# Attention, expert layer and gated layer on one core: expert stage and last stage in one block, idle matmuls in three waits of TensorE, and broadcasts of 1/rms behind the value share

## The chip, the cores and the metric

One core of one Trainium2 chip runs the whole program. Times are device microseconds of that core; a kernel's time is the median of its runs. TensorE, VectorE, ScalarE and GpSimd compute, SyncE (SP) issues the DMAs.

## The reference

```python
x = attention(q, k, v)              # 4 batches x 8 heads, 1152 queries pooled in pairs to 576, d 64
x = x.reshape(2304, 512)            # tokens
# expert layer with soft slots, 8 experts x 4 slots
logits = x @ phi                    # 2304 x 32
d = softmax(logits, over tokens);   slot_input = d.T @ x          # 32 x 512
slot_out[e] = relu(slot_input[e] @ w1[e]) @ w2[e]                 # 512 -> 1024 -> 512
c = softmax(logits, over slots);    x = c @ slot_out
# gated layer
xn = x / rms(x) * rms_g
out = (silu(xn @ w_gate) * (xn @ w_val)) @ w_out                  # 512 -> 1536 -> 512
```

All of it is fp32. The kernel never builds the x that enters the gated layer. It multiplies the 32 rows of `slot_out` by `w_gate` and `w_val` first (a share each of 32 x 1536) and then the softmax weights `c` by that. The factor 1/rms of each token is applied behind.

## The kernel before, in words

The program is four blocks one after another: attention, the routing of tokens to slots, the experts, the last stage. In a block each engine has its own list of instructions with semaphore waits written by hand; at the end of a block every engine, SP too, drains and meets the others.

**Routing** (lines 831 to 993). TensorE transposes x (L867), forms the logits (L877), transposes them back (L883, L886) and then waits for `col_exp`, the exponentials of the softmax over tokens: VectorE's maxima, one reduction over partitions by GpSimd, a subtraction by VectorE, the exponential by ScalarE (L918). Then come the weighted sums of x into `z_ps` (L892), the copy to `z_sum` (L922), a small product (L899) and `slot_in` (L988). VectorE prepares the inverse column sums meanwhile (L985).

**Experts** (lines 996 to 1188). Two groups of four experts, each expert in its own quarter of TensorE's columns. For a group: 32 matmuls into `h_ps` (L1103), relu by ScalarE, eight transposes, copies into `hid_t`, 32 matmuls into `o_ps` (L1139), a copy to `so_sb` (L1164), four transposes into `st_ps` (L1147), copies into `st_plain` (L1179) and, once, `st_scaled` (L1184). SP loads the second group's weights during the first: part c of `w1` when the part it overwrites has been used (`w1_used`, L1066), the four parts of `w2` behind (L1074), then `w_gv`, the weights of gate and value (L1079, L1081), and, when the second `o_ps` is complete, `w_out` into `wo_raw` in three issues (L1085). In the second group TensorE waits before every eighth of the 32 output matmuls for a part of `w2` (`w2_in[0]` to `w2_in[3]`). `stack_transposes` (L1034) writes the transposed softmax weights through `tb2`, and ScalarE copies them out (L1044, `ct_out`).

**Last stage** (lines 1193 to 1563). TensorE forms the Gram matrix of `st_plain` (L1304), ScalarE and VectorE split it into `gram_hi` and `gram`, TensorE multiplies the tokens by it (L1312, 20 matmuls of 32 columns), and VectorE and ScalarE make 1/rms from that (`inv_ready`). `share(m, c)` (L1259) adds part c to the share of gate (m = 0) or value (m = 1); `high_half` on ScalarE and `low_half` on VectorE split a share in two; `stack_share(k)` (L1273, L1275) puts quarter k of the eight into `tb3`, from which VectorE (even k) and ScalarE (odd k) copy it to `w_low`. `broadcast_inverse(n)` (L1282, L1287) spreads 1/rms of one batch (n = 0 to 3) or of the tails (4) over the partitions, in the PSUM bank `INV_BANK[n]`, and ScalarE copies it out (`inverse_out`, `bcast_out`). `gate` and `value` (L1296, L1300) make one tile of 128 hidden columns for 512 tokens; VectorE scales, ScalarE applies Silu (L1402), VectorE multiplies, and the product is split into `h_hi` (L1449) and `h_lo` (L1541). The loop over 5 chunks of tokens and 12 hidden tiles multiplies with the split `w_out` (L1364, three products per tile of tokens). `wo_hi` is made by ScalarE (L1381) and `wo_lo` by GpSimd (L1461), tile by tile ahead of the first chunk. The order of shares, broadcasts, gates and values ahead of this loop is written out by hand on TensorE and again on ScalarE (L1315 to L1345, L1404 to L1420). The accumulators `y_ps` of the loop are banks 4 to 7, so TensorE waits there for all broadcasts to be copied.

Of the kernel before, what the change touches and what calls it, by code (L numbers as in the profile page):

```python
# [6 lines left out]
P = 128  # L7
FP32 = mybir.dt.float32
F32R = mybir.dt.float32r
ALU = mybir.AluOpType  # L10
# [5 lines left out]
SQ = S // 2  # L16
# [745 lines left out]
def rest(nc, mem, phi, w1, w2, w_gate, w_val, w_out, rms_g, out):  # L762
# [95 lines left out]
    def _(pe):  # L858
# [28 lines left out]

        pe.wait_ge(col_exp, 1)
# [121 lines left out]
    tb2 = mem.ps("tb2", [P, 2, 512])  # L1010
# [44 lines left out]

    block = mem.block()
# [29 lines left out]

    @block.tensor
    def _(pe):
        for g in range(NG):
# [60 lines left out]
    @block.scalar  # L1150
    def _(act):
        for g in range(NG):
            act.wait_ge(h_ready, 2 * g + 1)
            if g:
                act.wait_ge(st_ready, g)
            nc.scalar.activation(hid[:, 0:512], h_ps[:, 0, :], ACT.Relu).then_inc(h_out, 1)
            act.wait_ge(h_ready, 2 * g + 2)
            nc.scalar.activation(hid[:, 512:1024], h_ps[:, 1, :], ACT.Relu).then_inc(h_out, 1)

            act.wait_ge(t_ready, 2 * g + 2)  # L1160
            if g:
                stack_out(act, tb2, plain_t)
            act.wait_ge(o_ready, g + 1)
            nc.scalar.copy(so_sb[:, 0:512], o_ps[:, :]).then_inc(o_out, 1)  # L1164

    @block.vector
    def _(dve):
        split_comb(dve)
        build_spread()
        for g in range(NG):  # L1170
            for n in range(2):
                dve.wait_ge(t_ready, 2 * g + n + 1)
                if g:
                    dve.wait_ge(o_ready, g)
                nc.vector.tensor_copy(hid_t[:, 4 * n:4 * n + 4, :],
                                      t_ps[:, n, :].rearrange("p (f q) -> p f q", f=4)).then_inc(t_out, 1)
            dve.wait_ge(st_ready, g + 1)
            for rep in range(4):
                last = nc.vector.tensor_copy(  # L1179
                    st_plain[:, :, rep, 16 * g:16 * g + 16].rearrange("p c (r s) -> p c r s", r=4),  # L1180
                    st_ps[:, :].rearrange("p (c r s) -> p c r s", c=KT, r=4)[:, :, :, 0:SPE])
            last.then_inc(st_out, 1)
        dve.wait_ge(st_out, NG)
        nc.vector.tensor_tensor(st_scaled[:], st_plain[:, :, 0, :],  # L1184
                                g_sb[:, :].unsqueeze(2).broadcast_to([P, KT, NS]), ALU.mult).then_inc(st_out, 1)
        dve.wait_ge(st_out, NG + 1)

    mem.end_block()

    mem.phase = mem.new_phase()
    QW = FF // 4
    N = NF * P
    CHUNKS = B + 1
    mem.at = r2
    w_low = mem.sb("w_low", [P, 2, FF], F32R)
    inv_rms = mem.sb("inv_rms", [P, NTOK], FP32)
    w_hi = mem.sb("w_hi", [P, 2, QW], F32R)  # L1200
    w_lo = mem.sb("w_lo", [P, 2, QW], F32R)
    assert mem.at <= r2 + 2 * SLOT
    mem.at = r2 + 4 * SLOT
    wo_hi = mem.sb("wo_hi", [P, NFT, DM], F32R)
    wo_lo = mem.sb("wo_lo", [P, NFT, DM], F32R)
    assert mem.at <= r3
    mem.at = r3
    scaled = mem.sb("scaled", [P, 2, N], FP32)
    silu = mem.sb("silu", [P, 2, N], FP32)
    hid2 = mem.sb("hid2", [P, 2, N], FP32)  # L1210
    h_hi = mem.sb("h_hi", [P, 3, N], F32R)
    h_lo = mem.sb("h_lo", [P, 3, N], F32R)
    y_sb = mem.sb("y_sb", [P, NF, DM], FP32)
    assert mem.at <= end_r3
    warm = hid[:, DM:DM + 2]

    banks = mem.ps("banks", [P, 8, 512])
    gv_ps = banks[:, 0:4, :].rearrange("p (f m) n -> p f m n", f=2)
    y_ps = banks[:, 4:8, :]
    g_ps = banks[:, 0, 0:NS]  # L1220
    gy_ps = banks[:, 2:4, :]
    w_ps = banks[:, 4:6, :]
    tb3 = banks[:, 6:8, :]
    INV_BANK = (1, 3, 4, 5, 4)

    gram_ready, gram_step, gy_ready = sem("gram_ready"), sem("gram_step"), sem("gy_ready")
    sq_step, mean_done, root, inv_ready = sem("sq_step"), sem("mean_done"), sem("root"), sem("inv_ready")
    bcast_ready, bcast_out = sem("bcast_ready"), sem("bcast_out")
    share_ready, share_hi, share_lo = sem("share_ready"), sem("share_hi"), sem("share_lo")
    wl_ready, wl_out_v, wl_out_a = sem("wl_ready"), sem("wl_out_v"), sem("wl_out_a")  # L1230
    wo_split_hi, wo_split_lo = sem("wo_split_hi"), sem("wo_split_lo")
    gate_ready, val_ready = sem("gate_ready"), sem("val_ready")
    scaled_done, silu_done, hid_done = sem("scaled_done"), sem("silu_done"), sem("hid_done")
    hi_done, lo_done, y_ready, y_out_a, y_out_v = sem("hi_done"), sem("lo_done"), sem("y_ready"), sem("y_out_a"), sem("y_out_v")
    used, stored, tail_done = sem("used"), sem("stored"), sem("tail_done")
    block = mem.block()
    SHARES = [(m, j) for m in range(2) for j in range(4)]

    def width_of(n):
        return N if n < B else TAIL * B  # L1240

    def columns(n):
        return slice(N * n, N * n + width_of(n))

    def tiles_of(n):
        return width_of(n) // P

    def row_scale(n, t):
        return tok_a[:, B * t + n:B * t + n + 1] if n < B else tail_inv[:, t:t + 1]

    def shares_out_before(k):
        return (k + 1) // 2, k // 2

    @block.tensor
    def _(pe):
# [83 lines left out]
        stack_share(6)  # L1339
        pe.wait_ge(bcast_out, 3)  # L1340
        broadcast_inverse(4)
        stack_share(7)
# [29 lines left out]
    def _(act):  # L1372

# [37 lines left out]
        inverse_out(1)  # L1411
        gate_silu(0)
        gate_silu(1)
        inverse_out(2)
        high_half(1)
        share_out(5)
        inverse_out(3)
        wo_high((0,))
        inverse_out(4)
# [21 lines left out]
        for n in range(CHUNKS):  # L1441
            width = width_of(n)
            for f in range(NFT):
# [22 lines left out]
    def _(dve):  # L1466
        dve.wait_ge(gram_step, 1)
# [79 lines left out]

    @block.sync
    def _(sp):
        o_rows = out.rearrange("(b s) d -> b s d", b=B)  # L1550
        o_full = o_rows[:, 0:NF * P, :].rearrange("b (p i) d -> p b (i d)", i=NF)
        for n in range(B):
            sp.wait_ge(y_out_a, 2 * n + 2)
            sp.wait_ge(y_out_v, 2 * n + 2)
            sp.dma_start(o_full[:, n, :], y_sb[:, :, :].rearrange("p i d -> p (i d)")).then_inc(stored, 16)
        sp.wait_ge(y_out_a, 2 * B + 1)
        sp.wait_ge(y_out_v, 2 * B + 1)
        for b in range(B):
            rows = slice(TAIL * (b % 2), TAIL * (b % 2) + TAIL)
            sp.dma_start(o_rows[b, NF * P:SQ, :], y_sb[rows, b // 2, :]).then_inc(stored, 16)  # L1560
        sp.wait_ge(stored, 16 * (2 * B))
# [84 lines left out]
```

## Time and profile before

| | |
|---|---|
| median of 3 runs | 858.87 us (858.35 to 860.64) |
| the profiled execution's own time | 856.21 us |
| its span | 854.4 us |
| TensorE busy | 792.5 us (93%) |
| VectorE busy | 497.3 us (58%) |
| ScalarE busy | 462.2 us (54%) |
| mean granted TensorE clock | 0.98 of 2.4 GHz |
| moved by DMA | 114.39 MB |

A row of the timeline is the start in us, the duration, the engine, the line and operation, result and operands, shape and the number of records; in brackets stand the idle time before it and what ended it. An fp32 matmul stands as two records. A row of the windows is the stretch, its length, the busy time of TensorE (or of each engine), the granted clock as a share of 2.4 GHz, the DMA engines' busy share and the GB/s they moved. Overlapping records are merged in busy times.

### The profile page before, as it was taken

The numbers are of one execution on the slowest core, as the hardware profiler recorded it, in microseconds if no ns is written. First come the engines' busy times: TensorE is split into PE (matmuls) and PEld (weight loads), VectorE is DVE, ScalarE is ACT, GpSimd is POOL, SyncE is SP. The second block draws the span as 40 slices with busy tenths as digits, with TensorE's granted clock in tenths as the row PEclk, the third lists the DMA queues.
The fourth block names the chain that finished last, engine by engine and source line by source line (L and its number), as shares of the span: only waits on it lengthen the run. The fifth ranks groups of instructions, "written<-read, shape, count | busy, mean of one in ns | idle before, by whom it ended". The sixth has DMA issues, their size and how long they took to land. (4 is left out here: it accounts for less than half of the span.)

```text
span 854.4 us, 17186 instructions
## 1 busy us (share of the span) xinstructions
PE 792.5 (93%) x5701; PEld 603.7 (71%) x5701; DVE 497.3 (58%) x956; ACT 462.2 (54%) x888; POOL 171.2 (20%) x230
## 2 busy tenths in 40 slices
PE   1799999999999999999999999986956899999997
PEld 1677777777778777777777777762314688888885
DVE  3566666576676566666665766645101566666664
ACT  1566666666667667666676666621112554334332
POOL 1323314314224124133143130000000240000000
PEclk9999999999999999999999999998986999999999
DMA  8984383473563653743734529346997001010111
GB/s 215 285 196 99 98 195 79 117 172 77 138 144 81 162 111 90 186 95 98 191 78 117 138 53 290 130 166 238 401 399 290 2 0 50 1 51 0 50 50 25
DMA packets 86328, 114.39 MB, mean 134 GB/s; under 512 B 48144, under 2 KB 50192, under 8 KB 85776
## 3 DMA queue, kind: packets, MB, share of 16 engines
q1 hardware_dynamic: 85488, 112.68, 46.7%
q10 hardware_dynamic: 800, 1.18, 0.6%
q8 instruction: 24, 0.39, 0.2%
q14 instruction: 16, 0.13, 0.0%
HBM read 71.37 MB, written 4.72 MB: 89 GB/s over the span
## 5 line engine op out<-in xcount | busy, mean ns | idle before, releaser
L490 PE MATMUL scores<-k_stack,q_stack 128*128 128x384 f32 x960 | 276.1, 377 | 15.2 <-DMA q_stack<-q_lo 14.7
L438 PE MATMUL tbank<-ident,probs 128*128 128x128 f32 x1296 | 220.0, 279 | 2.8 <-DVE pt L737 2.4
L639 ACT COPY pt<-tbank 128x384 f32<-128x384 f32 x256 | 122.7, 479 | 142.9 <-PE tbank L438 141.7
L438 PEld LDWEIGHTS tbank<-ident,probs 128*128 128x128 f32 x1296 | 156.6, 140 | 59.2 <-issue 42.7
L611 ACT ACTIVATE probs<-scores,neg_max 128x1152 f32<-128x1152 f32 x144 | 175.8, 1221 | 23.8 <-DVE neg_max L686 17.2
L490 PEld LDWEIGHTS scores<-k_stack,q_stack 128*128 128x128 f32 x960 | 148.8, 192 | 16.9 <-DMA q_stack<-q_lo 15.6
L682 DVE TENSOR_REDUCE row_max<-scores 128x1 f32<-128x384 f32 x144 | 80.1, 556 | 130.3 <-PE scores L490 128.4
L525 PE MATMUL obank<-pt,v_in 128*64 128x256 f32 x1152 | 148.8, 389 | 0.0
L675 DVE TENSOR_REDUCE row_max<-scores 128x1 f32<-128x768 f32 x144 | 136.7, 949 | 15.7 <-PE scores L490 12.8
L525 PEld LDWEIGHTS obank<-pt,v_in 128*64 128x64 f32 x1152 | 72.8, 136 | 49.3 <-issue 23.5
L323 POOL TENSOR_TENSOR k_hi<-k_lo,one 128x512 fp32r<-128x512 f32 (+1 forms) x45 | 37.2, 826 | 302.5 <-ACT k_lo L567 281.6
L737 DVE COPY pt<-tbank 128x384 f32<-128x384 f32 x128 | 71.3, 557 | 32.4 <-PE tbank L438 29.2
L1449 ACT CAST h_hi<-hid 128x512 fp32r<-128x512 f32 (+1 forms) x60 | 34.7, 578 | 99.3 <-DVE hid L1536 99.3
L1364 PE MATMUL banks<-wo_hi,h_hi 128*128 128x512 f32 x216 | 85.2, 395 | 1.1 <-DVE h_lo L1541 0.8
L1364 PE MATMUL banks<-wo_lo,h_hi 128*128 128x512 f32 x216 | 84.2, 390 | 0.0
L1364 PE MATMUL banks<-wo_hi,h_lo 128*128 128x512 f32 x216 | 84.1, 390 | 0.0
L1541 DVE TENSOR_TENSOR h_lo<-hid,h_hi 128x512 fp32r<-128x512 f32 (+1 forms) x60 | 38.3, 639 | 39.9 <-ACT h_hi L1449 39.9
L1500 DVE TENSOR_TENSOR scaled<-banks,inv_rms 128x512 f32<-128x512 f32 (+1 forms) x60 | 38.1, 636 | 24.7 <-PE banks L1296 24.7
L1364 PEld LDWEIGHTS banks<-wo_hi,h_hi 128*128 128x128 f32 x216 | 40.5, 188 | 12.1 <-DVE h_lo L1541 3.3
L1364 PEld LDWEIGHTS banks<-wo_hi,h_lo 128*128 128x128 f32 x216 | 40.6, 188 | 8.6
L1364 PEld LDWEIGHTS banks<-wo_lo,h_hi 128*128 128x128 f32 x216 | 40.6, 188 | 7.9
L328 POOL TENSOR_TENSOR k_lo<-k_lo,k_hi 128x512 fp32r<-128x512 f32 (+1 forms) x45 | 45.2, 1005 | 3.5
(159 smaller groups left out, 749.5 us busy)
## 6 DMA issues: line engine op xcount, KB each, us to landing
weights<-in_moe_w SPq DMA_DIRECT2D x7, 2048.0 KB, 10.6
k_in<-in_k SPq DMA_DIRECT2D x32, 288.0 KB, 4.7
v_in<-in_v SPq DMA_DIRECT2D x16, 576.0 KB, 3.9
k_stack<-k_hi SPq DMA_DIRECT2D x31, 288.0 KB, 4.0
k_stack<-k_lo SPq DMA_DIRECT2D x31, 288.0 KB, 3.7
q_in<-in_q SPq DMA_DIRECT2D x16, 512.0 KB, 5.0
slots_of_four<-in_moe_w SPq DMA_DIRECT2D x3, 2048.0 KB, 11.5
weights<-in_moe_w SPq DMA_DIRECT2D x12, 512.0 KB, 11.1
```

Source lines behind the costliest of these rows:

```text
L328: last = ops.tensor_tensor(low[:, cols], low[:, cols].bitcast(FP32), high[:, cols].bitcast(FP32), ALU.subtract)
L438: last = nc.tensor.transpose(tbank[:, bank, cols], src, ident[0:rows, 0:rows])
L490: last = nc.tensor.matmul(scores[:, bank, 0:CH], q_stack[at.par][:, h, order, cols], k_stack[at.par][:, h, keys], start=(x == 0), stop=(x ...
L525: last = nc.tensor.matmul(obank[rows, cols], v_in[:, par, h, D * kt:D * kt + D], rhs, start=(kt == 0), stop=(kt == NK - 1))
L611: nc.scalar.activation(probs[:, odd, :].rearrange("p (c k) -> p c k", c=3), scores[:, first:first + 3, 0:CH], ACT.Exp, bias=neg_max[:, odd ...
L639: nc.scalar.copy(pt_out(at, e), tbank[:, bank_of(at, e), 0:3 * P].rearrange("p (r q) -> p r q", r=3)).then_inc(out_by_act, 1)
L675: nc.vector.tensor_reduce(row_max[:, odd, 0:1], scores[:, first:first + 2, 0:CH], axis=AX.XY, op=ALU.max).then_inc(partial_max, 1)
L682: nc.vector.tensor_reduce(row_max[:, odd, 1:2], scores[:, 2, 0:CH], axis=AX.X, op=ALU.max).then_inc(partial_max, 1)
L737: nc.vector.tensor_copy(pt_out(at, e), tbank[:, bank_of(at, e), 0:3 * P].rearrange("p (r q) -> p r q", r=3)).then_inc(out_by_dve, 1)
L1364: last = nc.tensor.matmul(y_ps[:, t, :], a[:, f % 3, cols], w[:, f, :], start=(f == 0 and x == 0), stop=(f == NFT - 1 and x == 2))
L1500: nc.vector.tensor_tensor(scaled[:, f % 2, 0:width], gv_ps[:, f % 2, 0, 0:width], inv_rms[:, columns(n)], ALU.mult).then_inc(scaled_done, 1)
L1541: nc.vector.tensor_tensor(h_lo[:, f % 3, 0:width], hid2[:, f % 2, 0:width], h_hi[:, f % 3, 0:width].bitcast(FP32), ALU.subtract).then_inc( ...
```

## The change

Three edits.

1. The block boundary between experts and last stage goes. All PSUM of both is one tile `banks` of eight banks; `h_ps`, `t_ps`, `o_ps`, `st_ps` and `tb2` are views of banks 0 to 7, beside the views that the last stage had. The lists of the engines are joined: the code of the last stage stands, otherwise unchanged, behind that of the experts in each engine. TensorE waits for `st_out` (NG + 1) ahead of the Gram product and for `ct_out` ahead of L1312.
2. Idle matmuls, whose results nobody reads: four of 128x512 fp32 ahead of the wait for `col_exp`, and three ahead of each of the waits for `w2_in[2]` and `w2_in[3]` (`keep_clock`).
3. Broadcasts 1 and 2 move on TensorE from between the parts of the value share to behind it, broadcast 3 and 4 behind stack shares 6 and 7; the banks become (1, 4, 5, 4, 5). ScalarE's order follows.

```diff
@@ routing, TensorE
         nc.tensor.transpose(l_ps[0:TAIL, 1, 0:P], logit_t[:, NF * P:SQ], ident[:]).then_inc(l_ready, 1)
 
+        for _ in range(4):
+            nc.tensor.matmul(tb[:, NTB - 1, :], ident[:], x_nat[:, 0:NF * P], start=True, stop=True)
         pe.wait_ge(col_exp, 1)
@@ PSUM
-    h_ps = mem.ps("h_ps", [P, 2, 512])
-    t_ps = mem.ps("t_ps", [P, 2, 512])
-    o_ps = mem.ps("o_ps", [P, 512])
-    st_ps = mem.ps("st_ps", [P, 512])
+    banks = mem.ps("banks", [P, 8, 512])
+    h_ps, t_ps, o_ps, st_ps, tb2 = banks[:, 0:2], banks[:, 2:4], banks[:, 4], banks[:, 5], banks[:, 6:8]
-    tb2 = mem.ps("tb2", [P, 2, 512])
-    INV_BANK = (1, 3, 4, 5, 4)
+    INV_BANK = (1, 4, 5, 4, 5)
@@ experts, TensorE
+        def keep_clock(times):
+            pe.wait_ge(ct_out, len(ct_jobs))
+            for _ in range(times):
+                nc.tensor.matmul(tb2[:, 0, :], ident[:], hid_t[:, 0:4, :].rearrange("p f q -> p (f q)"),
+                                 start=True, stop=True)
                 if g and f % 2 == 0:
+                    if f >= 4:
+                        keep_clock(3)
                     pe.wait_ge(w2_in[f // 2], 64)
@@ end of the experts
-    mem.end_block()
-    mem.phase = mem.new_phase()
@@ last stage, TensorE
+        pe.wait_ge(st_out, NG + 1)
         for c in range(KT):
             last = nc.tensor.matmul(g_ps, st_plain[:, c, :, :].rearrange("p a s -> p (a s)"), st_plain[:, c, 0, :],
                                     start=(c == 0), stop=(c == KT - 1))
         last.then_inc(gram_ready, 1)
         pe.wait_ge(gram_step, 2)
+        pe.wait_ge(ct_out, len(ct_jobs))
...
         broadcast_inverse(0)
         share(1, 0)
+        share(1, 1)
         stack_share(2)
         stack_share(3)
-        broadcast_inverse(1)
-        share(1, 1)
         pe.wait_ge(wl_out_v, 1)
         gate(0, 0)
         gate(0, 1)
-        broadcast_inverse(2)
         share(1, 2)
         share(1, 3)
+        broadcast_inverse(1)
         stack_share(4)
         stack_share(5)
-        broadcast_inverse(3)
         pe.wait_ge(wl_out_v, 3)
-        pe.wait_ge(bcast_out, 2)
+        pe.wait_ge(bcast_out, 1)
         value(0, 0)
         value(0, 1)
+        broadcast_inverse(2)
         stack_share(6)
-        pe.wait_ge(bcast_out, 3)
-        broadcast_inverse(4)
+        pe.wait_ge(bcast_out, 2)
+        broadcast_inverse(3)
         stack_share(7)
+        pe.wait_ge(bcast_out, 3)
+        broadcast_inverse(4)
         pe.wait_ge(bcast_out, 5)
@@ last stage, ScalarE
         share_out(3)
-        inverse_out(1)
         gate_silu(0)
         gate_silu(1)
-        inverse_out(2)
         high_half(1)
+        inverse_out(1)
         share_out(5)
-        inverse_out(3)
         wo_high((0,))
-        inverse_out(4)
+        inverse_out(2)
+        inverse_out(3)
         share_out(7)
...
                 nc.scalar.copy(h_hi[:, f % 3, 0:width], hid2[:, f % 2, 0:width]).then_inc(hi_done, 1)
+                if k == 0:
+                    inverse_out(4)
                 if n == 0 and f + 1 < NFT:
                     wo_high((f + 1,))
```

## Rows read from the trace of the kernel before

**Rows 1.** The page, the span in 40 slices: granted clock of TensorE.

```profile
PEclk9999999999999999999999999998986999999999
```

**Rows 2.** Timeline of TensorE, 563 to 601 us.

```profile
563.35 8.32 PE L867 MATMUL tb<-ident,x_nat 128*128 128x128 f32 x80 [0.66 <-PEq L1598]
...
582.29 6.00 PE L892 MATMUL tb<-x_nat,exp_l 128*32 128x512 f32 x40 [4.47 <-ACT exp_l L918]
588.99 1.08 PE L899 MATMUL tb<-fold,z_sum 128*128 128x32 f32 x8 [0.71 <-ACT z_sum L922]
591.46 8.77 PE L1103 MATMUL h_ps<-weights,slot_in 128*32 128x512 f32 x64 [1.39 <-PEq L1598]
```

**Rows 3.** Windows: stretch, length, busy, granted clock, DMA share, GB/s.

```profile
560.00:580.00 20.00, 15.46 (x190) 12.06 (x190) 11.51 (x24) 5.76 (x12) 0.00 (x0) 1.00 0.44 138
...
630.00:640.00 10.00, 7.06 (x36) 1.71 (x36) 0.26 (x2) 0.58 (x1) 0.00 (x0) 0.67 1.04 410
...
585.00:586.00 1.00, 1.00 (x16) 0.95 1.01 414
591.00:592.00 1.00, 0.54 (x8) 0.96 0.00 0
595.00:596.00 1.00, 1.00 (x12) 0.83 0.17 57
656.00:657.00 1.00, 1.00 (x12) 0.61 0.27 92
```

**Rows 4.** Timeline of SP's issues, 590 to 650 us.

```profile
594.74 4.20 SPq L1066 DMA_DIRECT2D slots_of_four<-in_moe_w  x3
...
628.32 3.17 SPq L1081 DMA_DIRECT2D w_gv<-in_moe_w_val  x4
637.94 8.29 SPq L1085 DMA_DIRECT2D wo_raw<-in_moe_w_out  x3
```

**Rows 5.** Timeline of TensorE, 609 to 640 us.

```profile
609.52 0.66 PE L1147 MATMUL st_ps<-ident,hid 128*128 128x128 f32 x4 [0.76 <-ACT hid L1164]
...
624.35 1.92 PE L1139 MATMUL o_ps<-weights,hid_t 128*32 128x512 f32 x16 [0.98 <-DMA weights<-in_moe_w]
629.93 3.36 PE L1139 MATMUL o_ps<-weights,hid_t 128*32 128x512 f32 x16 [3.66 <-DMA weights<-in_moe_w]
635.24 2.66 PE L1139 MATMUL o_ps<-weights,hid_t 128*32 128x512 f32 x16 [1.95 <-DMA weights<-in_moe_w]
638.59 1.11 PE L1147 MATMUL st_ps<-ident,hid 128*128 128x128 f32 x4 [0.69 <-ACT hid L1164]
```

**Rows 6.** Timelines of VectorE and TensorE, ends of the two blocks.

```profile
587.41 0.35 DVE L985 RECIPROCAL col_a<-col_a 128x32 f32<-128x32 f32 x1
...
640.39 0.29 DVE L1184 TENSOR_TENSOR st_scaled<-st_plain,g_sb 128x128 f32<-128x128 f32 x1
...
646.67 1.89 PE L1304 MATMUL banks<-st_plain 128*128 128x32 f32 x8 [6.97 <-PEq L1598]
```

**Rows 7.** DMA issues, 555 to 720 us: count, KB each, median us to landing.

```profile
w_gv<-in_moe_w_val SPq DMA_DIRECT2D x4, 768.0 KB, 17.9
```

**Rows 8.** Timelines of TensorE, ScalarE and again TensorE, 649 to 675 us.

```profile
649.12 4.45 PE L1312 MATMUL banks<-gram,plain_t 128*128 128x32 f32 x20 [0.56 <-DVE gram L1469]
...
669.26 1.05 PE L1282 MATMUL banks<-ident,tok_a 128*128 128x128 f32 x8
...
665.48 1.23 ACT L1402 ACTIVATE silu<-scaled 128x512 f32<-128x512 f32 x2 [1.35 <-DVE scaled L1500]
667.34 0.48 ACT L1394 CAST w_hi<-banks 128x384 fp32r<-128x384 f32 x1 [0.16 <-PE banks L1259]
...
670.84 0.62 ACT L1381 CAST wo_hi<-wo_raw 128x512 fp32r<-128x512 f32 x1
672.74 0.48 ACT L1386 CAST w_low<-banks 128x384 fp32r<-128x384 f32 x1 [0.18 <-PE banks L1275]
...
674.61 0.47 PE L1364 MATMUL banks<-wo_hi,h_hi 128*128 128x512 f32 x1 [0.43 <-DVE h_lo L1541]
```

More of the change, by code:

```diff
@@ L1054, in build_spread @@
         nc.vector.memset(plain_t[:, NTOK:].bitcast(FP32), 0.0)
+    QW = FF // 4
+    N = NF * P
+    CHUNKS = B + 1
+    mem.at = r2
+    w_low = mem.sb("w_low", [P, 2, FF], F32R)
+    inv_rms = mem.sb("inv_rms", [P, NTOK], FP32)
+    w_hi = mem.sb("w_hi", [P, 2, QW], F32R)
+    w_lo = mem.sb("w_lo", [P, 2, QW], F32R)
+    assert mem.at <= r2 + 2 * SLOT
+    mem.at = r2 + 4 * SLOT
+    wo_hi = mem.sb("wo_hi", [P, NFT, DM], F32R)
+    wo_lo = mem.sb("wo_lo", [P, NFT, DM], F32R)
+    assert mem.at <= r3
@@ new lines, in rest @@
+    mem.at = r3
+    scaled = mem.sb("scaled", [P, 2, N], FP32)
+    silu = mem.sb("silu", [P, 2, N], FP32)
+    hid2 = mem.sb("hid2", [P, 2, N], FP32)
+    h_hi = mem.sb("h_hi", [P, 3, N], F32R)
+    h_lo = mem.sb("h_lo", [P, 3, N], F32R)
+    y_sb = mem.sb("y_sb", [P, NF, DM], FP32)
+    assert mem.at <= end_r3
+    warm = hid[:, DM:DM + 2]
+    gv_ps = banks[:, 0:4, :].rearrange("p (f m) n -> p f m n", f=2)
+    y_ps = banks[:, 4:8, :]
+    g_ps = banks[:, 0, 0:NS]
+    gy_ps = banks[:, 2:4, :]
@@ new lines, in rest, with width_of @@
+    wo_split_hi, wo_split_lo = sem("wo_split_hi"), sem("wo_split_lo")
+    gate_ready, val_ready = sem("gate_ready"), sem("val_ready")
+    scaled_done, silu_done, hid_done = sem("scaled_done"), sem("silu_done"), sem("hid_done")
+    hi_done, lo_done, y_ready, y_out_a, y_out_v = sem("hi_done"), sem("lo_done"), sem("y_ready"), sem("y_out_a"), sem("y_out_v")
+    used, stored, tail_done = sem("used"), sem("stored"), sem("tail_done")
+    SHARES = [(m, j) for m in range(2) for j in range(4)]
+    def width_of(n):
+        return N if n < B else TAIL * B
@@ L1056, in rest, with columns, tiles_of, row_scale @@
+    def columns(n):
+        return slice(N * n, N * n + width_of(n))
+    def tiles_of(n):
+        return width_of(n) // P
+    def row_scale(n, t):
+        return tok_a[:, B * t + n:B * t + n + 1] if n < B else tail_inv[:, t:t + 1]
+    def shares_out_before(k):
+        return (k + 1) // 2, k // 2
     block = mem.block()
@@ L1085, in _ @@
             sp.dma_start(wo_raw[:, 4 * n:4 * n + 4, :], wo_v[:, 4 * n:4 * n + 4, :]).then_inc(wo_in[n], 16)
+        o_rows = out.rearrange("(b s) d -> b s d", b=B)
+        o_full = o_rows[:, 0:NF * P, :].rearrange("b (p i) d -> p b (i d)", i=NF)
+        for n in range(B):
+            sp.wait_ge(y_out_a, 2 * n + 2)
+            sp.wait_ge(y_out_v, 2 * n + 2)
+            sp.dma_start(o_full[:, n, :], y_sb[:, :, :].rearrange("p i d -> p (i d)")).then_inc(stored, 16)
+        sp.wait_ge(y_out_a, 2 * B + 1)
+        sp.wait_ge(y_out_v, 2 * B + 1)
+        for b in range(B):
+            rows = slice(TAIL * (b % 2), TAIL * (b % 2) + TAIL)
+            sp.dma_start(o_rows[b, NF * P:SQ, :], y_sb[rows, b // 2, :]).then_inc(stored, 16)
+        sp.wait_ge(stored, 16 * (2 * B))
     @block.tensor
     def _(pe):
+        def keep_clock(times):
[3 more added lines that the diff above has]
+                                 start=True, stop=True)
         for g in range(NG):
@@ L1148, in _ @@
             last.then_inc(st_ready, 1)
[L1150 to L1186, printed above, removed]
@@ L1188, in rest @@
-    mem.end_block()
-    mem.phase = mem.new_phase()
[L1194 to L1221, printed above, removed]
@@ L1231, in rest @@
[L1231 to L1255, printed above, removed]
         def share(m, c):
@@ L1372, in _ @@
     def _(act):
+        for g in range(NG):
+            act.wait_ge(h_ready, 2 * g + 1)
+            if g:
+                act.wait_ge(st_ready, g)
+            nc.scalar.activation(hid[:, 0:512], h_ps[:, 0, :], ACT.Relu).then_inc(h_out, 1)
+            act.wait_ge(h_ready, 2 * g + 2)
+            nc.scalar.activation(hid[:, 512:1024], h_ps[:, 1, :], ACT.Relu).then_inc(h_out, 1)
+            act.wait_ge(t_ready, 2 * g + 2)
+            if g:
+                stack_out(act, tb2, plain_t)
+            act.wait_ge(o_ready, g + 1)
+            nc.scalar.copy(so_sb[:, 0:512], o_ps[:, :]).then_inc(o_out, 1)
         nc.scalar.activation(warm[:, 0:1], ident[:, 0:1], ACT.Sqrt)
@@ L1466, in _ @@
     def _(dve):
+        split_comb(dve)
+        build_spread()
+        for g in range(NG):
+            for n in range(2):
+                dve.wait_ge(t_ready, 2 * g + n + 1)
+                if g:
+                    dve.wait_ge(o_ready, g)
+                nc.vector.tensor_copy(hid_t[:, 4 * n:4 * n + 4, :],
+                                      t_ps[:, n, :].rearrange("p (f q) -> p f q", f=4)).then_inc(t_out, 1)
+            dve.wait_ge(st_ready, g + 1)
+            for rep in range(4):
+                last = nc.vector.tensor_copy(
+                    st_plain[:, :, rep, 16 * g:16 * g + 16].rearrange("p c (r s) -> p c r s", r=4),
+                    st_ps[:, :].rearrange("p (c r s) -> p c r s", c=KT, r=4)[:, :, :, 0:SPE])
+            last.then_inc(st_out, 1)
+        dve.wait_ge(st_out, NG)
+        nc.vector.tensor_tensor(st_scaled[:], st_plain[:, :, 0, :],
+                                g_sb[:, :].unsqueeze(2).broadcast_to([P, KT, NS]), ALU.mult).then_inc(st_out, 1)
+        dve.wait_ge(st_out, NG + 1)
         dve.wait_ge(gram_step, 1)
@@ L1546, in _ @@
         copy_out(CHUNKS - 1)
[L1548 to L1561, printed above, removed]
     mem.end_block()
```

22 lines of the change are left out of this document (11 added, 11 removed).

## The prediction

> **What bounds the kernel now.** I read the page first: TensorE's granted clock falls below full in slices 28 to 31 of 40, from 577 to 662 us [rows 1], where the three edits sit. Behind 674.61 us [rows 8] runs the main loop of the last stage, which the change does not touch; what is won ahead of it comes off the end one for one. So I walk the chain from 577 to 674.61 us and ask at each link what ends the wait.
>
> Link 1, column softmax. TensorE waits 4.47 us for the exponentials; the matmuls of `z_ps` then take 6.00 us, to 588.29 [rows 2]. The clock is a mean of full (1.00) and half (0.50) over a slice. It fell during the wait, and 0.95 in 585 to 586 puts the return at 585.10 [rows 3]: the first 2.81 us run at 1.2 GHz.
>
> Link 2, first expert group. L1103 starts at 591.46 [rows 2], falls to 1.2 GHz at 591.92 and is back at 595.34 [rows 3]. SP issues the next load of weights when the first 8 of its 32 matmuls (64 records) are done, at 594.74 [rows 4]. From there to 656.27 the 16 DMA engines are saturated (share 1.04 in 630 to 640, 0.27 in 656 to 657) [rows 3]. Loads are queued well ahead, so this stream moves as a whole with its first issue.
>
> Link 3, second expert group. The output matmuls come in groups of eight (16 records); the last three groups wait 0.98, 3.66 and 1.95 us, each for a DMA [rows 5]. The clock is low in most of 630 to 640 (0.67) [rows 3], so the last two take 3.36 and 2.66 us where the one before them, at full clock, takes 1.92 [rows 5].
>
> Link 4, the boundary between the blocks. VectorE's last instruction ends at 640.68, yet TensorE starts at 646.67 [rows 6]. What holds both is SP: its three issues of `wo_raw` begin at 637.94 and take 8.29 us, to 646.23 [rows 4]. Their data are first read at 670.84 [rows 8].
>
> Link 5, the start of the loop at 674.61, on `h_lo` [rows 8]. ScalarE copies the last share only at 672.74 and `h_hi` behind it. These queue behind the share of `val`, whose high half was taken at 667.34 [rows 8], because two broadcasts (L1282) stood ahead of it on TensorE.
>
> **The change part by part.**
>
> Idle matmuls in the wait for `exp_l`: four of 128x512 fp32, not in the trace. From above: one broadcast is four matmuls of 128 columns in 1.05 us, tail included [rows 8], so 0.26 per 128 columns and 1.05 per 512. From below: a group of four column tiles of 512 in L1103, with its 3.42 us at half clock taken at half, is (8.77 - 1.71)/8 = 0.88 us [rows 2]. I take 0.88, the row of equal width: 3.5 us, 4.2 at most, inside the 4.47 us wait, which is the cover. If the cover went, they would cost what sticks out. They write a spare bank whose copy has been waited for, and nobody waits for them. If they hold the clock, 2.81 us at half rate become 1.41: gain **1.40**. The copy of `z_sum`, L899 and `slot_in` follow at once; the column sums are ready at 587.76 [rows 6], before the new `slot_in` at 588.78. L1103 starts at 590.06.
>
> The stream's start. Old, the 8 matmuls had 0.46 us at full clock and 2.82 at half, 1.87 us of full-clock work. From 590.06 that ends at 591.93, just as the clock fell in this trace, so they run full: 594.74 becomes 591.93, of which **1.41** beyond the 1.40. Bounds: 0 if the clock falls ahead of them, 1.9 if they had been slow throughout and become fast. I take the value of this trace. The issues behind keep a backlog, so the two loads that link 3 waits for come 2.81 earlier.
>
> Idle matmuls in the waits for `w2_in[2]` and `w2_in[3]`: three each, 2.65 us (3.15 at most). First wait 3.66: covered. Second: the group before it now takes 1.92, not 3.36, so the wait is 635.24 - 631.85 = 3.39: covered by 0.24 at the worst. The first of these groups gains nothing, since the next load ends the wait anyway; the last gains 2.66 - 1.92 = **0.74**. Their wait on `ct_out` is for copies that run under the first output group, and costs nothing. The four transposes behind take 1.11 us; in the first expert group, at full clock, 0.66 [rows 5]: **0.45**.
>
> One block. L1304 now waits for `st_scaled` alone: 640.68 plus 0.05 instead of 646.67, **5.94**. Queued behind TensorE's new waits (`st_out`, `ct_out`) is the Gram product, which needs both in any case. SP goes on issuing behind it; its next work, the output store, is some 60 us off. ScalarE's table load for Sqrt moves behind its copy of `so_sb`, under transposes and copies. The shared bank views add no instruction. Are the next loads there? `val` is issued by 631.5 [rows 4] and lands a median 17.9 us on [rows 7]; the stream ends at 656.3. New needs, even if the stream did not move: the first share at about 646.5, the last of `val` at about 657, `wo_hi` at about 661. The gates are issued ahead of `val`, and a mere 0.3 us beyond the first share's need would show as a wait there.
>
> The order of the broadcasts. Two of them leave the path ahead of the share of `val`, which then ends about 1.9 us earlier. But ScalarE still does both Silu first, a pair of 1.23 us [rows 8], which ends at 665.83 in the old frame: high half then, not at 667.34, 1.51 earlier. Then on TensorE shares 4 and 5 (to 667.75), a wait for VectorE's copy, the values (to 668.85), broadcast 2, share 6, broadcast 3, share 7 (671.4), broadcast 4 (672.4). ScalarE: share 7 at 671.7 instead of 672.74, `h_hi` 672.2, the last broadcast copy to 673.1, for which the loop's first gate waits: with gate and value, 0.25 us each, the loop starts at 673.65. Gain **0.95**; bounds 0, if ScalarE's order gives it all back, and 1.5, if the high half alone counted. Behind the moved copies is `wo_hi` of the second tile and GpSimd's subtraction; the loop wants it a group of twelve products later.
>
> Sum: 1.40 + 1.41 + 0.74 + 0.45 + 5.94 + 0.95 = 10.9 us. The mean product L1312 (4.45 us at half clock [rows 8]) and the shares stay as they are. Against the profiled execution's 856.21 that gives 845.3. The median shown, 858.87, is 2.66 above it, so the forecast for the median is **848.0 us**. About 0.3% (2.6 us) is what a measurement of this kernel can tell from no change.
>
> **The rule weighed.** L867 is 8.32 us of transposes [rows 2], and the clock is 1.00 over 560 to 580 [rows 3]: transposes held it. The Trainium skill, page "TensorE: Matmul & The Clock Gate", Part 4, says that a transpose does not count as busy for the gate. By that rule the clock is lost at the transposes behind the last expert group, whatever the idle matmuls did, and the sum stays 10.9; by the row it may be held, rival A. The trace disagrees with the rule at L867.
>
> **The rivals.**
> - A, the clock holds across the merged boundary (25%). For: the transposes above; the gap behind them shrinks from 6.97 us [rows 6] to one. Against: 20 products of 32 columns in a row ran at half clock to their end. Price: L1304 from 1.89 to 1.08, as L899 of the same shape [rows 2], and L1312 at best halved, 4.45 to 2.2: up to 3.0, so 845.0.
> - B, the stream does not start earlier (17%). The clock falls ahead of the first 8 matmuls, or the early stream is waited for elsewhere; both 1.40 and 1.41 are lost. For: before this fall stood a product of 32 columns and two waits, which the idle matmuls leave alone. Gain 8.1: 850.8.
> - C, slower (3%). The idle matmuls themselves run at half clock, 1.77 us each. Four end at 584.9, 2.6 late, and the loads with them; the next three end 1.7 later still, the group behind takes 3.8, three more 5.3, the last group 3.8: `o_ready` 9.5 later, against 6.9 won by boundary and order. 2.6 slower: 861.5. It decides once the lateness passes 6.9. Against: the clock reads 1.00 where each wait begins.
> - D, something besides SP holds the start of the last stage (5%), such as a first share that waits for its gates once it comes early. Half of the 5.94 goes: 851.
> The forecast has the other 50%, with its own range of 846.5 to 849.5.
>
> **How the numbers follow.** The range reaches past A with half of its price again, 843.5, and past B and D, 852.0. Slower by over 0.3% is C, 0.03; a remainder in which B, D and a part of C meet is the same, 0.02; the rest is faster, 0.95.
>
> **What would show it.** Right: `z_ps` in about 4.6 us; SP's first issue of expert weights near 592; L1304 within 0.1 us of `st_scaled`, near 637; loop start near 664. Wrong: an idle matmul that ends after the wait it sits in; L1304 later than 639; a DMA as the releaser of a share; a loop start behind 667.

## The result, and the profile after

| | before | after |
|---|---|---|
| median | 858.61 us (4 runs, 858.17 to 860.64) | 845.36 us (4 runs, 844.40 to 847.90) |
| profiled execution | 856.21 us | 844.80 us |
| its span | 854.4 us | 842.9 us |
| mean granted clock | 0.98 | 0.995 |

The ratio of after to before is 0.9846, 95% interval 0.9818 to 0.9873: 13.2 us less, between 10.9 and 15.6. Forecast were 10.9 us and 848.0, in the range 843.5 to 852.0. The two profiled executions differ by 11.4. The four signs that the prediction named for being right all came: `z_ps` in 4.63 us, SP's first issue at 592.69, the Gram product 0.05 us behind `st_scaled` (637.50), the loop at 663.09.

Timeline of TensorE in the changed kernel, from the softmax wait to the first product of the loop. The columns are those of [rows 2].

```profile
578.13 0.27 PE L886 MATMUL tb<-ident,logit_t 128*64 128x128 f32 x1
578.24 3.60 PE L889 MATMUL tb<-x_nat,ident 128*128 128x512 f32 x8
582.91 4.63 PE L894 MATMUL tb<-x_nat,exp_l 128*32 128x512 f32 x40 [1.08 <-ACT exp_l L920]
588.25 1.08 PE L901 MATMUL tb<-fold,z_sum 128*128 128x32 f32 x8 [0.70 <-ACT z_sum L924]
590.72 7.07 PE L1179 MATMUL banks<-weights,slot_in 128*32 128x512 f32 x64 [1.39 <-PEq L1592]
...
624.27 2.84 PE L1162 MATMUL banks<-hid_t,ident 128*128 128x512 f32 x6
627.83 1.92 PE L1217 MATMUL banks<-weights,hid_t 128*32 128x512 f32 x16 [0.72 <-DMA weights<-in_moe_w]
629.69 2.84 PE L1162 MATMUL banks<-hid_t,ident 128*128 128x512 f32 x6
633.23 1.92 PE L1217 MATMUL banks<-weights,hid_t 128*32 128x512 f32 x16 [0.70 <-DMA weights<-in_moe_w]
635.86 0.66 PE L1225 MATMUL banks<-ident,hid 128*128 128x128 f32 x4 [0.71 <-ACT hid L1360]
637.55 1.08 PE L1277 MATMUL banks<-st_plain 128*128 128x32 f32 x8 [1.04 <-DVE st_scaled L1472]
639.27 3.75 PE L1286 MATMUL banks<-gram,plain_t 128*128 128x32 f32 x20 [0.63 <-DVE gram L1478]
642.94 4.72 PE L1231 MATMUL banks<-w_gv,st_scaled 128*32 128x384 f32 x32
...
663.09 0.45 PE L1339 MATMUL banks<-wo_hi,h_hi 128*128 128x512 f32 x1
```

The idle matmuls (L889, L1162) end before the waits they sit in; the group of `z_ps` takes 4.63 us for 6.00 in [rows 2], the last two output groups 1.92 each for 3.36 and 2.66 in [rows 5]. L1277 is released by `st_scaled`, not by the boundary as in [rows 6], and runs at full clock. L1286 begins at full clock too, and loses it, as the windows show (stretch, length, busy, granted clock, DMA share, GB/s):

```profile
639.00:640.00 1.00, 0.73 (x7) 1.00 1.00 412
640.00:641.00 1.00, 1.00 (x7) 0.53 1.00 412
...
646.00:647.00 1.00, 1.00 (x12) 0.55 1.00 385
```

SP in the changed kernel, for [rows 4]:

```profile
592.69 3.80 SPq L1123 DMA_DIRECT2D slots_of_four<-in_moe_w  x3
...
635.22 9.00 SPq L1142 DMA_DIRECT2D wo_raw<-in_moe_w_out  x3
```

It still takes 9.00 us over `wo_raw`, to 644.22, and nobody waits for it any more.

Executions reach the softmax wait at different times, 577.8 to 580.5 us over all profiles here, and every edit sits behind that point. So I measure each landmark from the end of the last routing transpose (577.81 before, 578.40 after):

| from that point, us | before | after | difference of the step |
|---|---|---|---|
| SP's first expert issue | 16.93 | 14.29 | -2.64 |
| transposes behind the last output group start | 60.78 | 57.46 | -0.68 |
| Gram product starts | 68.86 | 59.15 | -6.39 |
| gate share starts | 75.69 | 64.54 | -1.44 |
| gate share ends | 80.08 | 69.26 | +0.33 |
| loop starts | 96.80 | 84.69 | -1.29 |
| end of span | 276.59 | 264.50 | +0.02 |

The steps add to 12.1; the 0.6 us by which this execution came later to the wait makes it 11.5, the difference of the spans.

### The profile page after: what moved, and what is told of

Its sections match the earlier page's. It is cut to its first block and busy times, and to the rows that moved or that the text cites. A ratio compares the mean times of both kernels' runs of the same rounds, so it can differ in the third digit from the quotient of the medians.

```text
span 842.9 us, 17216 instructions
## 1 busy us (share of the span) xinstructions
PE 793.8 (94%) x5721; PEld 603.5 (72%) x5721; DVE 497.6 (59%) x956; ACT 462.5 (55%) x888; POOL 171.4 (20%) x230
## 3 DMA queue, kind: packets, MB, share of 16 engines
HBM read 71.37 MB, written 4.72 MB: 90 GB/s over the span
## 5 line engine op out<-in xcount | busy, mean ns | idle before, releaser
L1339 PEld LDWEIGHTS banks<-wo_hi,h_hi 128*128 128x128 f32 x216 | 40.5, 188 | 11.5 <-DVE h_lo L1550 3.4
```

The lines of the kernel that those rows point to most:

```text
L1339: last = nc.tensor.matmul(y_ps[:, t, :], a[:, f % 3, cols], w[:, f, :], start=(f == 0 and x == 0), stop=(f == NFT - 1 and x == 2))
```

## The experiments

The first four kernels ran together with the kernel before on one chip, the next four on another, the last three on a third. Each median stands beside that of the kernel before in its own group: 859.85 (23 runs, 855.90 to 863.63), 858.36 (11 runs) and 859.77 (11 runs).

### The boundary alone

```diff
@@ the changed kernel, less idle matmuls and new order
-        for _ in range(4):
-            nc.tensor.matmul(tb[:, NTB - 1, :], ident[:], x_nat[:, 0:NF * P], start=True, stop=True)
-                    if f >= 4:
-                        keep_clock(3)
-    INV_BANK = (1, 4, 5, 4, 5)
+    INV_BANK = (1, 3, 4, 5, 4)
...
```

> The kernel before with the block boundary alone taken out. Theory 1: what held the last stage was SP, stuck in its three issues of wo_raw; without the barrier L1304's product starts within 0.1 us of st_scaled, 5.9 us earlier, at half clock as before, and nothing else moves: about 852.7 against 858.6. Theory 2: without the idle matmuls the early product meets weights that have not landed, and part of the 5.9 comes back as a DMA wait of the first share: 855 or more.

Measured: 853.77 us, ratio 0.9924 (0.9901 to 0.9946), that is 6.5 us less, between 4.6 and 8.5. ScalarE's and TensorE's order is that of before as well. Timeline of TensorE:

```profile
584.04 7.09 PE L892 MATMUL tb<-x_nat,exp_l 128*32 128x512 f32 x40 [4.47 <-ACT exp_l L918]
...
594.30 7.07 PE L1177 MATMUL banks<-weights,slot_in 128*32 128x512 f32 x64 [1.39 <-PEq L1586]
...
637.04 3.49 PE L1213 MATMUL banks<-weights,hid_t 128*32 128x512 f32 x16 [3.39 <-DMA weights<-in_moe_w]
641.24 0.66 PE L1221 MATMUL banks<-ident,hid 128*128 128x128 f32 x4 [0.72 <-ACT hid L1355]
642.94 1.29 PE L1273 MATMUL banks<-st_plain 128*128 128x32 f32 x8 [1.04 <-DVE st_scaled L1466]
644.86 4.45 PE L1282 MATMUL banks<-gram,plain_t 128*128 128x32 f32 x20 [0.63 <-DVE gram L1472]
```

Theory 1 holds: the product starts 0.06 us behind `st_scaled` (642.88), and from the last routing transpose to it are 63.37 us for 68.86, 5.5 less. One part of it fails: the product did not run at half clock as before, but took 1.29 us for 1.89, because the clock lay differently over the whole stretch (last output group 3.49 for 2.66, transposes 0.66 for 1.11, gate share 5.07 for 4.39). No share waits for a load. The trace also shows a thing that the trace of before did not: without idle matmuls `z_ps` can take 7.09 us, not 6.00, while L1177 then runs at full clock, 7.07, not 8.77. The sum of the two is about the same, 14.2 and 14.8; the half-clock stretches only fall differently.

### The issues of `wo_raw` behind the barrier

```diff
@@ the kernel before, SP
-        sp.wait_ge(o_ready, NG)
-        for n in range(3):
-            sp.dma_start(wo_raw[:, 4 * n:4 * n + 4, :], wo_v[:, 4 * n:4 * n + 4, :]).then_inc(wo_in[n], 16)
@@ last block, SP
+        wo_v = w_out.rearrange("(f p) n -> p f n", p=P)
+        for n in range(3):
+            sp.dma_start(wo_raw[:, 4 * n:4 * n + 4, :], wo_v[:, 4 * n:4 * n + 4, :]).then_inc(wo_in[n], 16)
         o_rows = out.rearrange("(b s) d -> b s d", b=B)
```

> The kernel before, with SP's three issues of wo_raw moved to the start of its list in the last block; the barrier stays. Theory 1: the barrier itself costs about 0.8 us (as at the end of the routing block), the rest of the 5.9 is the wait for the issues: 5.2 us less, about 853.4. Rival: the 5.9 is the meeting of the engines and their drains: at most 0.5 less, 858.

Measured: 854.25 us, ratio 0.9929 (0.9904 to 0.9953), 6.1 us less, between 4.0 and 8.3. The timelines of VectorE, TensorE and SP:

```profile
642.40 0.29 DVE L1181 TENSOR_TENSOR st_scaled<-st_plain,g_sb 128x128 f32<-128x128 f32 x1
...
643.22 1.65 PE L1301 MATMUL banks<-st_plain 128*128 128x32 f32 x8 [1.50 <-PEq L1598]
...
643.16 4.66 SPq L1549 DMA_DIRECT2D wo_raw<-in_moe_w_out  x3
```

The barrier is still there, yet the wait is 1.50 us and not 6.97; the product starts 0.53 us behind `st_scaled` (642.69). So of the 5.99 us that the boundary cost behind `st_scaled`, 5.5 were SP, stuck in issues for data that nobody needed, and 0.5 the meeting of the engines. The rival falls. Moving the issues wins nearly what the merged block wins: the loop starts 91.99 us behind the last routing transpose here and 91.47 with the boundary gone, for 96.80.

### The idle matmuls alone

```diff
@@ the kernel before, TensorE
+        for _ in range(4):
+            nc.tensor.matmul(tb[:, NTB - 1, :], ident[:], x_nat[:, 0:NF * P], start=True, stop=True)
         pe.wait_ge(col_exp, 1)
...
+                    if f >= 4:
+                        keep_clock(3)
                     pe.wait_ge(w2_in[f // 2], 64)
```

> The kernel before with the idle matmuls alone, four in the softmax wait and three in each of two waits for w2. Theory 1: the stream of weights starts 2.7 us earlier and the second o_ready comes 3.9 earlier, but the boundary waits for SP's issues, which are paced by the stream, so only the stream's 2.7 reach the end: about 855.9. Theory 2: the parts add up, 4 us or more: 854.6 or less. Theory 3: clock won in a stretch that waits for DMA anyway is worth nothing: 858.

Measured: 859.50 us, ratio 0.9975 (0.9952 to 0.9998): 2.1 us less, between 0.2 and 4.1. The medians show only 0.35; the runs of both kernels are spread widely (853.19 to 861.05 over these 12). The timelines of TensorE and SP tell where it goes:

```profile
635.44 1.92 PE L1149 MATMUL o_ps<-weights,hid_t 128*32 128x512 f32 x16 [0.69 <-DMA weights<-in_moe_w]
638.07 0.66 PE L1157 MATMUL st_ps<-ident,hid 128*128 128x128 f32 x4 [0.71 <-ACT hid L1174]
646.84 1.88 PE L1314 MATMUL banks<-st_plain 128*128 128x32 f32 x8 [8.11 <-PEq L1608]
...
653.65 5.35 PE L1269 MATMUL banks<-w_gv,st_scaled 128*32 128x384 f32 x32
...
637.42 8.97 SPq L1087 DMA_DIRECT2D wo_raw<-in_moe_w_out  x3
```

From the last routing transpose (580.49) the transposes start at 57.58, 3.2 earlier than before, but the Gram product at 66.35, only 2.5 earlier: the boundary wait has grown from 6.97 to 8.11, because SP's issues, paced by the stream, end at 646.39. Then the gate share takes 5.35 for 4.39, the clock coming back later in it. Of 3.2 us, 1.55 reach the loop. Theory 1 is right in the trace as far as the Gram product, 2.5 for 2.7, but not to the end, and the parts do not add up: the idle matmuls pay in full only with the boundary gone.

### The order alone

```diff
@@ the kernel before, TensorE (ScalarE's order likewise)
         broadcast_inverse(0)
         share(1, 0)
+        share(1, 1)
         stack_share(2)
         stack_share(3)
-        broadcast_inverse(1)
-        share(1, 1)
...
```

> The kernel before with the new order of broadcasts and their banks alone. Theory 1: 0.95 to 1.3 us from the last w_low copy and h_hi on ScalarE: about 857.5, and the loop start that much closer to the first share. Theory 2: ScalarE's own order gives it back: within 0.3 of 858.6.

Measured: 857.23 us, ratio 0.9975 (0.9956 to 0.9993), 2.1 us less, between 0.6 and 3.8. The trace:

```profile
655.05 5.35 PE L1259 MATMUL banks<-w_gv,st_scaled 128*32 128x384 f32 x32
...
675.83 0.44 PE L1365 MATMUL banks<-wo_hi,h_hi 128*128 128x512 f32 x1
```

The gate share ends at 660.40 and the loop starts at 675.83: 15.43 us from the one's end to the other's start. Before, it is 674.61 - 657.89 = 16.72; in the changed kernel 663.09 - 647.66 = 15.43 again. The order is worth 1.29 us, alone or with the rest.

### Without the softmax idle matmuls

```diff
@@ the changed kernel
-        for _ in range(4):
-            nc.tensor.matmul(tb[:, NTB - 1, :], ident[:], x_nat[:, 0:NF * P], start=True, stop=True)
         pe.wait_ge(col_exp, 1)
```

> The changed kernel without the four idle matmuls in the softmax wait. Theory 1: z_ps loses 1.4 us at half clock and the first expert part 1.3, and the whole stream of weights starts 2.7 later: about 848.1 against 845.4. Rival: the stream's start does not carry to the end, 1 us or less: under 846.4.

Measured: 847.37 us, ratio 0.9879 (0.9857 to 0.9901), against 0.9846 with them, on another chip: 2.8 us, though the two intervals overlap. The trace has, for SP and TensorE,

```profile
595.23 3.80 SPq L1121 DMA_DIRECT2D slots_of_four<-in_moe_w  x3
...
665.81 0.44 PE L1337 MATMUL banks<-wo_hi,h_hi 128*128 128x512 f32 x1
```

From the last routing transpose (578.31) SP's first issue is at 16.92, for 14.29, and the loop at 87.50, for 84.69: 2.63 at the stream's first issue, 2.81 at the loop. Theory 1 holds against this profile of the changed kernel; what starts the stream late reaches the end. Against the changed kernel's second profile, further below, which lost the clock in the first expert part, it is only 1.0 at the issue and 1.1 at the loop.

### Without the load idle matmuls

```diff
@@ the changed kernel
-                    if f >= 4:
-                        keep_clock(3)
                     pe.wait_ge(w2_in[f // 2], 64)
```

> The changed kernel without the idle matmuls in the two waits for w2. Theory 1: the last output group, the transposes and the products across the merged boundary go back to half clock, 0.74 + 0.45 + 1.1: about 847.7. Rival: only the last output group, 0.7: 846.1.

Measured: 849.37 us, ratio 0.9895 (0.9875 to 0.9916), 4.2 us above the changed kernel by the ratios, more than either theory. TensorE's timeline:

```profile
591.93 8.63 PE L1179 MATMUL banks<-weights,slot_in 128*32 128x512 f32 x64 [1.39 <-PEq L1590]
...
636.29 3.49 PE L1215 MATMUL banks<-weights,hid_t 128*32 128x512 f32 x16 [3.39 <-DMA weights<-in_moe_w]
640.50 0.66 PE L1223 MATMUL banks<-ident,hid 128*128 128x128 f32 x4 [0.71 <-ACT hid L1358]
642.19 1.29 PE L1275 MATMUL banks<-st_plain 128*128 128x32 f32 x8 [1.04 <-DVE st_scaled L1470]
644.12 4.45 PE L1284 MATMUL banks<-gram,plain_t 128*128 128x32 f32 x20 [0.64 <-DVE gram L1476]
```

The loop starts at 669.00, 89.39 behind the last routing transpose for 84.69: 4.7 us. 1.57 of it has nothing to do with the edit: L1179 lost the clock ahead of its start (8.63 for 7.07), although the softmax idle matmuls were there, and SP's first issue is at 15.86 for 14.29. The edit's own part is 3.1: the last output group wholly at half clock (3.49 for 1.92, where the trace of before had 2.66), the Gram product 0.21, L1284 0.70, the share 0.35, and a load that was waited for 0.3 later. The loss in L1179 is rival B's mechanism, the clock falling ahead of the first eight matmuls (at 591.72 here), but as a thing that some executions show and others don't.

### The softmax idle matmuls doubled

```diff
@@ the changed kernel
-        for _ in range(4):
+        for _ in range(8):
             nc.tensor.matmul(tb[:, NTB - 1, :], ident[:], x_nat[:, 0:NF * P], start=True, stop=True)
```

> The changed kernel with eight idle matmuls in the softmax wait instead of four. They take 7.2 us in a wait of 4.5. Theory 1: z_ps starts 2.5 us later than in the changed kernel and the whole chain with it, 0.90 us for each idle matmul that sticks out: about 847.9. Rival: DMA time further down absorbs it: under 846.4.

Measured: 849.97 us, ratio 0.9911 (0.9888 to 0.9935), 5.6 us above the changed kernel.

```profile
578.18 7.03 PE L889 MATMUL tb<-x_nat,ident 128*128 128x512 f32 x16
585.14 4.63 PE L894 MATMUL tb<-x_nat,exp_l 128*32 128x512 f32 x40
...
592.95 8.77 PE L1179 MATMUL banks<-weights,slot_in 128*32 128x512 f32 x64 [1.39 <-PEq L1592]
```

Eight take 7.03 us where four take 3.60, so one is (7.03 - 3.60)/4 = 0.86 us (forecast 0.88), and `z_ps` starts 6.80 behind the last transpose, for 4.51: 2.3 us late. Nothing further down absorbs that. In the profiled execution L1179 lost the clock too, 0.75 us behind its start: SP's first issue is 3.3 late (17.60 for 14.29), 1.0 of it from that, and the loop 4.5 (89.16 for 84.69), 1.3 of it from the Gram product to the end of the share at half clock (4.45 for 3.75, 5.14 for 4.72). So 2.3 us is the price of the overshoot, as expected within 0.2, and 2.2 more came with the clock in this execution. What the other five runs did was not seen.

### The gate share ahead of the mean product

```diff
@@ the changed kernel, last stage, TensorE
         last.then_inc(gram_ready, 1)
+        for c in range(KT):
+            share(0, c)
         pe.wait_ge(gram_step, 2)
...
-        for c in range(KT):
-            share(0, c)
         stack_share(0)
         stack_share(1)
-        pe.wait_ge(inv_ready, 1)
-        broadcast_inverse(0)
         share(1, 0)
         share(1, 1)
+        pe.wait_ge(inv_ready, 1)
+        broadcast_inverse(0)
@@ ScalarE
         nc.scalar.copy(gram_hi[:], g_ps).then_inc(gram_step, 1)
+        high_half(0)
+        share_out(1)
         act.wait_ge(mean_done, 1)
...
-        high_half(0)
-        share_out(1)
@@ VectorE: low_half(0) ahead of the wait for gy_ready, share_out(0) ahead of the wait for root
```

> The changed kernel with the four parts of the gate share ahead of the product of tokens and Gram matrix, so that ScalarE and VectorE split the share and make 1/rms under TensorE's work; the first broadcast comes behind two parts of the value share. If the start of the last stage is a chain of handovers between the engines and the loads are no bound, the 1.2 us wait for the low half and the 0.6 us wait for gram go, and the products run at full clock: 2 to 3 us less, about 843. Rival: the shares then wait for their loads, whose stream ends at a fixed time: within 1 us of 845.4, with a DMA as the releaser of a share.

Measured: 844.50 us, ratio 0.9833 (0.9807 to 0.9860); the profiled execution took 840.78. Its timeline of TensorE:

```profile
637.13 1.08 PE L1277 MATMUL banks<-st_plain 128*128 128x32 f32 x8 [1.04 <-DVE st_scaled L1472]
638.14 3.08 PE L1231 MATMUL banks<-w_gv,st_scaled 128*32 128x384 f32 x32
641.15 2.40 PE L1288 MATMUL banks<-gram,plain_t 128*128 128x32 f32 x20
643.40 0.42 PE L1245 MATMUL banks<-w_hi,spread 128*128 128x384 f32 x1
...
658.13 0.44 PE L1339 MATMUL banks<-wo_hi,h_hi 128*128 128x512 f32 x1
```

Both handover waits, 0.63 us for `gram` and 1.20 for `w_lo`, are gone (a new one of 0.42 us for 1/rms stands ahead of the first broadcast), and everything up to the loop runs at full clock: the share 3.08 us for 4.72, the mean product 2.40 for 3.75. The loop starts 80.19 behind the last routing transpose, 4.5 earlier than in the changed kernel, and no share waits for a load. But the runs showed only about 1 us, from another chip. So both went once more, together.

### Both again on one chip, and one idle matmul ahead of the experts

The first two are the kernels above, unaltered; the third adds one line.

> The changed kernel once more, beside the share-first version on one chip. Theory: 13 to 14 us below the kernel before. The first expert part (64 records into h_ps) takes 7.07 us when the clock is held and 8.6 to 8.8 when not, and which of the two it is changes from run to run; the second costs 1.6 us.

> The share-first version once more. Its trace put the loop 4.5 us earlier behind the last routing transpose than the changed kernel's, its median only 0.9 us lower on another chip. If the trace is right, it is 3.5 to 4.5 us below the changed kernel on the same chip; if the trace was a lucky one, 1 us.

```diff
@@ the share-first version, end of the routing block, TensorE
         last.then_inc(s_ready, 1)
+        nc.tensor.matmul(tb[:, NTB - 1, 0:256], ident[:], x_nat[:, 0:256], start=True, stop=True)
```

> The share-first version with one more idle matmul, 128x256 (0.43 us), behind the product that makes slot_in, where TensorE waits 1.4 us for the block boundary. If the clock lost ahead of the first expert part is what spreads the runs, that part takes 7.07 us in its profile and the median comes 0.5 to 1 us below the share-first version's; rival: the drain at the boundary waits for the idle matmul and it is 0.2 to 0.4 us slower.

| kernel | median, us | runs | ratio (95%) | L1179, us | loop start behind the last transpose |
|---|---|---|---|---|---|
| changed, again | 846.95 | 844.35 to 848.67 | 0.9846 (0.9821 to 0.9870) | 8.66 | 86.43 |
| share first, again | 844.00 | 842.87 to 844.41 | 0.9814 (0.9791 to 0.9838) | 8.77 | 82.60 |
| share first, idle matmul ahead of the experts | 841.41 | 841.00 to 845.95 | 0.9797 (0.9771 to 0.9823) | 7.07 | 80.17 |

The share-first version is 2.95 us below the changed kernel by the medians on one chip, 3.8 by the landmark: more than the 1 us of a lucky trace, and of the 3.5 to 4.5 expected otherwise the landmark shows as much, the medians a little less. Both profiled executions lost the clock at L1179, the changed kernel at 590.64, ahead of its start at 590.80, the share-first one at 591.34, behind its start at 591.07. In the windows of the share-first one,

```profile
590.00:591.00 1.00, 0.00 (x0) 1.00 0.20 82
591.00:592.00 1.00, 0.93 (x8) 0.67 0.03 12
592.00:593.00 1.00, 1.00 (x8) 0.50 0.00 0
```

and with the idle matmul ahead of the boundary (0.68 us in the trace, its tail included) the same stretch is

```profile
589.00:590.00 1.00, 1.00 (x7) 1.00 0.81 324
590.00:591.00 1.00, 0.12 (x5) 1.00 0.16 66
591.00:592.00 1.00, 1.00 (x12) 1.00 0.04 16
592.00:593.00 1.00, 1.00 (x14) 1.00 0.00 0
```

with L1180 at 7.07 us and the wait at the boundary shorter by just the idle matmul (0.88 for 1.39), so the drain does not wait for it. The median is 2.6 us lower, more than expected, 1.5 by the ratios, whose intervals overlap. By the landmark it is 2.4: 1.5 at SP's first issue, and 0.9 because the share-first execution lost the clock once more, at 645.96, behind the mean product, so that the value share ran at half clock:

```profile
646.73 2.77 PE L1231 MATMUL banks<-w_gv,st_scaled 128*32 128x384 f32 x16
```

It takes 1.50 us with the added idle matmul. That the idle matmul is the cause is not shown: the first profile of the share-first version held the clock without it, with the loop at 80.19. Nor can one profile say that the clock is now held in every execution (one of the six runs took 845.95). The direction is as expected. By the ratios that kernel is 2.0% below the kernel before and the best measured here.

## Why the prediction was right

**The softmax idle matmuls and the stream's start: 1.40 + 1.41 forecast, 2.64 measured** at SP's first issue, 2.8 when they are taken out. The mechanism and the price of an idle matmul (0.88 forecast, 0.86) are as put; cover held. The division between the two terms was a property of the one trace: in four profiles without them (boundary alone, order alone, `wo_raw` later, softmax idle out) `z_ps` takes 7.09 to 7.29 us and the first expert part 7.07, so there the whole gain lies in `z_ps`. Their sum, seen as SP's first issue, is 16.71 to 16.93 in all five. The column sums did not come late. That 2.64 came so near 2.81 is in part luck: of the six profiles with four idle matmuls and nothing ahead of the experts, three have that issue at 14.29 or 14.30, three at 15.80 to 15.89, and for these the two terms together are worth about 1 us.

**The last output group, 0.74 forecast, 0.68 with the wait's own shift.** Size right against this trace, small against others: without idle matmuls the group takes 3.49 to 3.64 us in four other profiles, so the usual gain is 1.6 to 1.7.

**Transposes 0.45 and boundary 5.94: 6.39 forecast, 6.39 measured.** That it was SP and not the barrier is shown by the run that moved its issues alone. With the boundary alone gone the same stretch, from the start of the transposes to the Gram product, is 1.70 us for 8.08, 6.38 less. So the 0.45 did not need the idle matmuls, to which the forecast gave it: in the four profiles without them in the load waits, other than that of before, the transposes take 0.66 us as well.

**The order, 0.95 forecast, 1.29 measured**, twice. The term was undersized by 0.34: by the old frame the loop was put 15.76 behind the gate share's end, and it is 15.43. The loop's first gate starts on the last broadcast copy, as forecast. What was off is a few tenths in the handovers ahead of it: behind the gate share's end the high half of the value share was put at 7.94 us and came at 7.79, and the last broadcast copy was to end at 15.21 and ended at 14.82.

**What the sum lacked.** L1304 and L1312 were left at half clock. They gained 0.81 and 0.70, with 0.07 lost in a gap, and the gate share lost 0.33, since the clock, fallen at 640.06, came back only at 646.90, 3.96 of its 4.72 us in (before, 3.28 of 4.39): 1.1 net. This is a third of rival A's 3.0. The share-first version has all of it: 1.08 and 2.40.

So the sum by the traces is 2.64 + 0.68 + 6.39 + 1.44 - 0.33 + 1.29 = 12.1 against 10.9. The rest up to 13.2 is the basis, traced only in part: the profile of before, 856.21, was one of the shortest executions. Over all groups the kernel before took 855.90 to 863.85. The forecast added the 2.66 us between it and the median but took the size of the clock's losses from it. One profile bears on that: with the order alone changed the loop starts at 96.27, which with its 1.29 put back is 97.56, 0.8 more than the 96.80 of before. In the other direction, the second profile of the changed kernel has the loop at 86.43, 10.4 earlier than before and not 12.1. How often either kernel loses the clock, and where, the medians do not tell.

**The rivals.** A came in part. B did not decide the result, but its mechanism is real: the first expert part ran partly at half clock in four of the seven profiles that have the softmax idle matmuls and nothing ahead of the experts, and in the three of them where nothing else ahead of it differed the stream started 1.5 to 1.6 us later for it. C did not come; the doubled run shows what an overshoot costs at full clock, 0.86 us for each idle matmul past the wait, not what C put, idle matmuls at half clock. D did not: no share waited for its gates, even when the share came first.

**The rule weighed.** Behind the last dense product (635.15) the changed kernel has four transposes, the Gram product and the first records of L1286 before the clock falls at 640.06. Whether the transposes helped to hold it so long, no run separates from the idle matmuls ahead of them. L867, 8.32 us at a granted clock of 1.00, remains the evidence against the rule that was weighed.

## What to carry to other kernels

Ask of a barrier which engine comes last and what that engine was doing: an issue into a saturated DMA stream held its sequencer for up to 6.57 us here, and work that only queues transfers for a later stage belongs behind the barrier, or the barrier away. Idle matmuls paid here where the clock's loss sat ahead of the issues that pace a saturated stream (0.8 to 2.6 us), and behind the last load that ends a wait (3.1 us), and only as far as they end inside the wait; size them by one measured record and recount when the wait changes. Measure such edits by landmarks in the trace from a common point: the runs of one kernel spread by 1.5 to 7.9 us and left a term of 1.29 us between 0.6 and 3.8, while two traces agreed on it to the hundredth. But one trace shows one draw of the clock; take two before a gain of 1 to 2 us is put down to an edit.

## What the runs showed of the hardware

- SP's three issues of `wo_raw`, 1 MB each, took 0.38, 1.97 and 6.57 us one after another in the changed kernel, all in a stream at some 410 GB/s (ns, shortest, median and longest):

```profile
L1142 SPq DMA_DIRECT2D wo_raw<-in_moe_w_out x3: 378/1966/6568, 635.2 to 637.6; - x3
```

  So a saturated stream does not hold every issue, but the later ones. That SP was held was read from the trace of before; that of the 6.0 us at the barrier 5.5 were this and 0.5 the barrier, against the 0.8 expected for it, was not.
- The 20 products of the tokens with the Gram matrix took 4.45 us at half clock and 2.40 at full. In the changed kernel the granted clock fell from 1.00 to 0.50 at 640.06, 0.79 us into them, and they took 3.75. With the dense share of 3.08 us directly ahead they ran at full clock to their end; in one of these three profiles the clock fell 0.3 us behind them.
- The 4.47 us wait ahead of `z_ps` cost the clock in all five profiles without idle matmuls in it, but at different places: four lost 2.5 to 2.7 us in `z_ps` (7.09 to 7.29 for 4.63), one lost 1.4 there and 1.7 in the first expert part (8.77 for 7.07). A single trace shows one of these.
